# Retention attention and two expert layers on one core: one causal mask, another order of loads, and VectorE's sums moved at the seams

## What is computed

```python
# attention: q, k, v are (4, 8, 768, 64)
for t in range(S):
    state = gamma * state + outer(k[:, :, t], v[:, :, t])
    y[:, :, t] = scale * q[:, :, t] @ state
x = y.transpose(0, 2, 1, 3).reshape(3072, 512)
# first network, w_in 512 x 2048, w_out 2048 x 512
h = x @ w_in
x2 = where(h > 0, h, exp(min(h, 0)) - 1) @ w_out
# second network, w_in 512 x 1024, w_out 1024 x 512
h = x2 @ w_in2
sm = exp(h - max(h)) / (sum(exp(h - max(h))) + 1e-9)
solu = h * sm
out = ((solu - mean) / sqrt(var + 1e-6) * g_ln) @ w_out2
```

## Time and profile before

| | us |
|---|---|
| runs, median of 3 (lowest to highest) | 857.64 (855.99 to 858.91) |
| profiled execution | 856.04 |
| its span | 854.3 |
| TensorE busy in the span | 840.5 |
| VectorE, ScalarE, GpSimd busy | 553.7, 419.0, 390.1 |

### The profile page before, as it was taken

The page is one execution under the profiler, slowest core; times in us unless marked ns, Lnnn a source line. Parts: engine busy times, 40 slices in busy tenths (PEclk is TensorE's granted clock), DMA queues, the critical chain, the costliest instruction groups (busy, mean ns, idle before and its releaser), DMA issues.

```text
span 854.3 us, 12592 instructions
## 1 busy us (share of the span) xinstructions
PE 840.5 (98%) x4852; PEld 694.9 (81%) x4852; DVE 553.7 (65%) x848; ACT 419.0 (49%) x679; POOL 390.1 (46%) x446
## 2 busy tenths in 40 slices
PE   9997999999999999999999999999999999999998
PEld 6987788888888888888888888887878888888886
DVE  3585667677735455576345655788887777777773
ACT  4566665655525555544355565563333333333322
POOL 3577667575006657540256651464253343444200
PEclk9999999999999999999999999999999999999999
DMA  8999611013103001050111101613011111111001
GB/s 305 362 369 347 228 30 45 25 50 128 49 1 96 28 25 49 26 173 1 43 56 31 44 26 44 203 50 98 26 50 50 49 49 39 51 50 50 25 13 50
DMA packets 49359, 73.32 MB, mean 86 GB/s; under 512 B 3218, under 2 KB 23954, under 8 KB 49044
## 3 DMA queue, kind: packets, MB, share of 16 engines
q1 hardware_dynamic: 48864, 72.43, 25.2%
q10 hardware_dynamic: 436, 0.08, 0.0%
HBM read 55.73 MB, written 16.78 MB: 85 GB/s over the span
## 4 chain that ended last, share of the span: by engine, by line
PE 92%; DVE 4%; ACT 1%; issue 1%; POOL 1%; DVEq 0%; ACTq 0%; POOLq 0%
PE ps L673 10%; PE ps L677 10%; PE ps L674 10%; PE ps L626 9%; PE ps L628 9%; PE ps L627 9%; PE ps L783 5%; PE ps L785 5%; PE ps L784 5%; PE ps L685 4%; PE ps L687 4%; PE ps L686 4%; PE ps L576 3%; PE ps L603 3%; PE ps L769 2%; PE ps L589 1%
## 5 line engine op out<-in xcount | busy, mean ns | idle before, releaser
L494 POOL TENSOR_TENSOR u_lo<-u_raw,u_hi 128x256 fp32r<-128x256 f32 x168 | 142.0, 878 | 193.5 <-ACT u_hi L1117 193.5
L673 PE MATMUL ps<-g_hi,wd_hi 128*128 128x512 f32 x384 | 149.4, 389 | 0.0
L674 PE MATMUL ps<-g_hi,wd_lo 128*128 128x512 f32 x384 | 149.4, 389 | 0.0
L677 PE MATMUL ps<-g_lo,wd_hi 128*128 128x512 f32 x384 | 149.4, 389 | 0.0
L626 PE MATMUL ps<-x_hi,u_hi 128*128 128x512 f32 x336 | 131.3, 391 | 1.2 <-DVE u L888 1.2
L627 PE MATMUL ps<-x_hi,u_lo 128*128 128x512 f32 x336 | 130.8, 389 | 0.0
L628 PE MATMUL ps<-x_lo,u_hi 128*128 128x512 f32 x336 | 130.7, 389 | 0.0
L489 POOL TENSOR_TENSOR u_raw<-u_raw 128x256 f32<-128x256 f32 x96 | 88.7, 923 | 17.3 <-DMA u_raw<-w_dram 11.1
L677 PEld LDWEIGHTS ps<-g_lo,wd_hi 128*128 128x128 f32 x384 | 72.1, 188 | 15.0
L674 PEld LDWEIGHTS ps<-g_hi,wd_lo 128*128 128x128 f32 x384 | 72.1, 188 | 15.0
L673 PEld LDWEIGHTS ps<-g_hi,wd_hi 128*128 128x128 f32 x384 | 72.1, 188 | 14.9
(11 more groups left out here) (91 smaller groups left out, 1498.1 us busy)
## 6 DMA issues: line engine op xcount, KB each, us to landing
u_raw<-w_dram SPq DMA_DIRECT2D x24, 512.0 KB, 3.5
k<-units_dram SPq DMA_DIRECT2D x12, 512.0 KB, 6.4
q<-units_dram SPq DMA_DIRECT2D x12, 512.0 KB, 4.8
v<-units_dram SPq DMA_DIRECT2D x12, 512.0 KB, 7.3
x_between<-x SPq DMA_DIRECT2D x24, 256.0 KB, 2.7
x_raw<-x_between SPq DMA_DIRECT2D x12, 512.0 KB, 3.5
out_dram<-y_sb SPq DMA_DIRECT2D x24, 256.0 KB, 2.0
kn<-units_dram SPq DMA_DIRECT2D x10, 512.0 KB, 6.1
```

What stands on the lines that cost most here:

```text
L494: nc.gpsimd.tensor_tensor(u_lo[n % 2][:, o, :], u_raw[n % 2][:, o, :], u_hi[n % 2][:, o, :].bitcast(f32), ALU.subtract).then_inc(ul_done, 1)
L673: nc.tensor.matmul(ps[:, bank + m, :], hi, g_hi[:, no % 3, :], start=(f == 0), stop=False)
L674: nc.tensor.matmul(ps[:, bank + m, :], lo, g_hi[:, no % 3, :], start=False, stop=False)
L677: last = nc.tensor.matmul(ps[:, bank + m, :], hi, g_lo[:, no % 3, :], start=False, stop=(f == NF1 - 1))
```

## The change

1. q is multiplied by its decay in every step. `mask0`, the three row products, the copies out of them and their semaphores are gone; `apply_mask` always takes the causal table. VectorE multiplies the two chunks of q in S0, GpSimd those of all later steps, S6 included.
2. The decay of q comes as a table of 256 KB, first on SyncE's queue; the 7 KB load of rows on ScalarE's queue goes.
3. `load_step(s)` loads q, v, k and natural k of step s, all behind one wait for the attention of step s-3.
4. 13 products on zeros ahead of the first scores, not 6.
5. First network: in pair 0, VectorE's u3 comes ahead of the activation of the first quadrant and the first split of the second weight; u2 of pair 1 comes ahead of pair 0's last activation.
6. Second network: `solu_moments` is cut in two, `solu_spread` and `solu_variance`. u2 of the second pair comes ahead of both for tile 0, u3 ahead of the product of tile 1; u3 of the third pair comes between the two parts of tile 3. For the last pair the maximum of the last tile comes behind the variance of the tile before.

```diff
-WARM = 6
+WARM = 13
             def load_step(s):
-                step_over(s - SLOTS)
+                if s >= SLOTS:
+                    sp.wait_ge(att_done, s - SLOTS + 1)
+                load(s, q_sb, 0, q_in)
                 load(s, v_sb, 3, v_in)
-                if s + 1 < NS:
-                    step_over(s + 1 - SLOTS)
-                    load(s + 1, q_sb, 0, q_in)
+                load(s, k_sb, 1, k_in)
                 if s % NC < NC - 1:
                     load(s, kn_sb, 2, kn_in)
-                if s + 1 < NS:
-                    load(s + 1, k_sb, 1, k_in)
...
-            load(0, k_sb, 1, k_in)
-            load(0, q_sb, 0, q_in)
+            sp.dma_start(q_decay[:, :], tables[:, T_QDEC:T_QDEC + HH * C]).then_inc(q_decay_in, 16)
...
-                if (s + 1) % NC > 0:
+                if s + 1 < NS:
                     decay_q(s + 1)
...
             def scores(s):
-                if s % NC > 0:
-                    pe.wait_ge(q_decayed, decays(s))
-                else:
-                    pe.wait_ge(q_in[slot], 16 * loads(s))
+                if s > 0:
+                    pe.wait_ge(q_decayed, s)
                 for one in range(2):
-                    if s > 0:
+                    if s == 0:
+                        pe.wait_ge(q0_decayed, one + 1)
+                    else:
                         pe.wait_ge(masked, 2 * s - 1 + one)
...
-            spread_row(0, 4)
-            spread_row(1, 5)
...
-                table = causal[:, :].unsqueeze(1).to_broadcast([P, H, C]) if s % NC else mask0
+                table = causal[:, :].unsqueeze(1).to_broadcast([P, H, C])
...
+            dve.wait_ge(q_decay_in, 16)
+            dve.wait_ge(q_in[0], 16)
+            for one in range(2):
+                nc.vector.tensor_tensor(q_sb[0][:, one, :], q_sb[0][:, one, :], q_decay[:, :], ALU.mult)\
+                    .then_inc(q0_decayed, 1)
...
-                dve.wait_ge(p1_kept, n + 1)
-                keep_sum(u2[:, :], n, U2, h21, Y, M6)
-                activate(e11, n, G11, X)
-                if blk == 0:
-                    wd_split_lo(2 * i)
+                if n != 1:
+                    keep_u2(n)
+                if n > 0:
+                    activate(e11, n, G11, X)
+                    if blk == 0:
+                        wd_split_lo(2 * i)
                 keep_sum(u3[:, :], n, U3, h21, Y, M7)
+                if n == 0:
+                    activate(e11, n, G11, X)
+                    wd_split_lo(0)
...
+                if n == 0:
+                    keep_u2(1)
                 activate(stash[:, 2 * i, :], n, G12, stash[:, 2 * i, :])
...
             solu_product(0)
-            solu_moments(0)
             dve.wait_ge(p1_copied, 2)
             add(u2[:, :], 1, U2, kept, Y, P6)
+            solu_spread(0)
+            solu_variance(0)
             solu_normalise(0)
+            add(u3[:, :], 1, U3, kept, Y, P7)
             solu_product(1)
-            add(u3[:, :], 1, U3, kept, Y, P7)
...
-                solu_max(t + 3)
+                if not final:
+                    solu_max(t + 3)
                 solu_product(t + 2)
-                solu_moments(t + 2)
+                solu_spread(t + 2)
+                solu_variance(t + 2)
+                if final:
+                    solu_max(t + 3)
                 solu_normalise(t + 2)
```

More of the change, by code:

```diff
@@ L48, with build @@
 TILE_OF = {place_of(n): n for n in range(NCH)}
-def build(nc, units, w1, w_in2, w_out2, g_ln, tables, rows_table, x_dram, x2_dram, out):
+def build(nc, units, w1, w_in2, w_out2, g_ln, tables, x_dram, x2_dram, out):
     f32, f32r = mybir.dt.float32, mybir.dt.float32r
@@ L863, in split_x_lo @@
                 nc.vector.tensor_tensor(x_lo[:, o], x_raw[:, o], x_hi[:, o].bitcast(f32), ALU.subtract).then_inc(xl_done, 1)
-            for s in range(NS):
[L866 to L874, removed]
+            dve.wait_ge(q_decay_in, 16)
[3 more added lines that the diff above has]
+                    .then_inc(q0_decayed, 1)
+            dve.wait_ge(causal_in, 16)
+            for s in range(NS):
                 apply_mask(s, 0)
@@ L1002, in solu_product, with solu_spread @@
                 nc.vector.tensor_tensor(e3[:, par, :], e3[:, par, :], h2[:, par, :], ALU.mult).then_inc(soft[par], 1)
-            def solu_moments(t):
+            def solu_spread(t):
                 u, par, done = t // 2, t % 2, soft[t % 2]
                 z = SOFT * u
-                esum, esum_eps, r, r2, v = (column(t, n) for n in (2, 3, 4, 5, 7))
+                esum, esum_eps, r = (column(t, n) for n in (2, 3, 4))
                 nc.vector.tensor_scalar(esum_eps, esum, EPS_SM, None, ALU.add).then_inc(done, 1)
@@ L1012, in solu_moments, with solu_variance @@
                     nc.vector.bn_stats(bn[par][:, 6 * q:6 * q + 6], e3[:, par, 512 * q:512 * q + 512]).then_inc(done, 1)
+            def solu_variance(t):
+                u, par, done = t // 2, t % 2, soft[t % 2]
+                z = SOFT * u
+                r, r2, v = (column(t, n) for n in (4, 5, 7))
                 dve.wait_ge(done, z + 7)
@@ L1036, in _ @@
             solu_product(0)
[L1037 removed]
             dve.wait_ge(p1_copied, 2)
             add(u2[:, :], 1, U2, kept, Y, P6)
+            solu_spread(0)
+            solu_variance(0)
             solu_normalise(0)
+            add(u3[:, :], 1, U3, kept, Y, P7)
             solu_product(1)
[L1042 to L1043 removed]
+            dve.wait_ge(soft[1], 3)
             add(h2[:, 1, 512:1024], 1, H22, u3[:, :], W, P5)
             normalised_lo(0)
[L1046 removed]
+            solu_spread(1)
+            solu_variance(1)
             add(h2[:, 1, 0:512], 1, H21, kept, Y, P4)
@@ L1134, in _ @@
             decay_v(0)
-            act.wait_ge(spread, 3)
-            nc.scalar.activation(q_decay[:, :], ps[:, 7, :], ACT.Copy).then_inc(q_decay_made, 1)
             for s in range(NS):
@@ L1319, in decay_tables @@
     state_decay = np.tile(gamma[head] ** C, (1, 2))
-    q_rows = (scale * gamma[:, None] ** (t + 1)[None, :]).reshape(2, HH * C)
-    first, second = np.eye(2)
-    both = np.arange(P) // D == np.arange(2)[:, None]
-    rows = [q_rows, np.tile(first[:, None], (1, P)), np.tile(second[:, None], (1, P)), both]
-    return (np.concatenate([causal, np.eye(P), v_decay, state_decay], axis=1).astype(np.float32),
-            np.concatenate(rows, axis=1).astype(np.float32))
+    q_decay = scale * gamma[head][:, :, None] ** (t + 1)[None, None, :]
+    parts = [q_decay.reshape(P, HH * C), causal, np.eye(P), v_decay, state_decay]
+    return np.concatenate(parts, axis=1).astype(np.float32)
 def kernel(q, k, v, moe_w_in, moe_w_out, moe2_w_in, moe2_w_out, moe2_g_ln):
@@ L1343 @@
         moe_w_out.reshape(NF1, P, DM).transpose(1, 0, 2)], axis=1)
-    tables, rows_table = decay_tables()
     arrays = {
@@ L1350 @@
         "g_ln": np.ascontiguousarray(moe2_g_ln.reshape(NF2, P).T),
-        "tables": tables,
-        "rows": rows_table,
+        "tables": decay_tables(),
     }
```

37 lines of the change are left out of this document (12 added, 25 removed).

## The result

| | before | changed |
|---|---|---|
| median of 8 runs each, us (lowest to highest) | 855.64 (852.47 to 858.91) | 848.18 (846.25 to 849.54) |
| profiled execution, us | 856.04 | 846.25 |
| its span | 854.3 | 844.5 |

The ratio of the runs is 0.9911, with a 95% interval from 0.9890 to 0.9932: the change takes 7.5 us off. The forecast was 850.5, in a range from 846.0 to 855.5. The profiled execution of the change is the fastest of its eight and that of before lies a little above its median, so the two traces differ by 9.8 us and not by 7.5. How much of that is the start's own spread is part of what follows.

What follows compares the result with a forecast made beforehand. TensorE was taken as the bound, its chain stretched or broken in places. From 856.04 us, -3.7 - 1.75 - 0.4 - 0.2 = -6.05 gave 850.0; 0.5 added for the median made 850.5 us, range 846.0 to 855.5.

Steps and rivals of the forecast that it cites:

- The bound: Whole kernel: TensorE is busy 840.5 of 854.3 us; gains lie only where its chain is stretched or broken.
- Term 1: Start of attention: first step at full clock rate, second step starting at 14.3 and not 18.05 us; -3.7 us.
- That the 13 products make the clock: Before the first scores: 13 bf16 products raise TensorE's clock in time; rival, not raised: 853.0 us, chance 0.17.
- Term 2: Attention stalls with each step's loads behind one wait: 3.6 us lost instead of 5.35; -1.75 us, bounds -5.35 and +4.55.
- 1 us lost in S1 and S2 together: Second and third attention steps: instruction blocks stand behind the deep starting queue of loads, about 1 us lost.
- 2.6 us in S8 to S10: Ninth to eleventh attention steps: 2.6 us still lost, as u loads and stores of x still crowd in.
- blocks never late: Rival on the attention stalls: with loads better ordered all 5.35 us go, giving 846.4 us; chance 0.17.
- v late: Tenth attention step, ahead of values: v landing late delayed ScalarE's copy; the 1.29 us break should go.
- The first seam: First network, pairs 0 and 1: VectorE's sums earlier, TensorE then waits for ScalarE's p; -0.4 us, between 0 and -1.2.
- The second seam: Second network: VectorE's sums moved ahead of the statistics delay the normalisation as much; 0, between +0.7 and -1.5 us.
- The last pair: Second network, last pair: last tile's maximum moves behind the variance of the tile before; -0.2 us, between 0 and -0.8.

## Why the prediction was right, and where its terms were not

The direction, the range and the place of the gain were right. By its own steps:

- **The bound.** TensorE's chain, stretched at the start, broken at the end of attention and at the seams. Right: every saving lies there, and nothing moved in between.
- **Term 1, the start, -3.7.** S0 came at 8.24 to 9.57 in three profiles (forecast 9.1), S1 at 13.4 to 15.6 (forecast 14.3). Against the one profile of before that is -2.4 to -4.5. But before's own start was not a constant: over the six profiles that begin as before did (all with the old loads but the one with natural k early, which has 18.72), S1 starts at 15.07 to 17.98, 16.7 on average; over three that begin as the change does (its two, and the one with 17 products), at 14.6. The term is nearer to -2.1, an estimate from few and scattered profiles. The step that failed is that S0's half rate was taken from one profile as the rule.
- **That the 13 products make the clock.** Right in the traces (2.06 against 3.79 us for the scores), though six were enough in two profiles of before, and one of the change lost the clock again in the pause. I priced its absence at 3.0 us, and it was 1.7 in S0, about 1 behind the waits for k, and less than the measurement can tell.
- **Term 2, the losses, -1.75.** This was the mis-sized term: 4.7 us went in the trace (5.34 to 0.66), and 4.7 by the ratio with the loads alone (3.0 to 6.5). "1 us lost in S1 and S2 together" was 0.75 in the first profile, but for k's loads and not for blocks, and nothing in the second; "2.6 us in S8 to S10" was nothing. I had reasoned that a deep queue of loads delays the block. The queue at the start was the deepest, and the block passed 3.3 us after TensorE entered the one before. The prediction also took 6.75 and 9.45 us, from one resumption to the next, as what a block takes; the 9.45 hold the wait for v of 1.29, and the packets themselves passed 4.2 and 7.2 us after TensorE entered the block before, with some 2.4 more until it resumed. And the three breaks stood 6, 5 and 3 matmuls into the group, not 5 to 7. The rival "blocks never late" was the true case there, and the sentence of the Trainium skill (*Runtime: NRT & Kernel Launch*, instruction fetch mechanics) that crossing a block is mostly hidden held for the new order, as it had not for the old.
- **v late.** Right, and larger than the 1.29 us that I gave it: in the old order v and natural k are late by turns.
- **The first seam, -0.4.** -0.5, and by the path forecast: TensorE now waits for ScalarE's p, 0.83 us.
- **The second seam, 0.** +0.3: the sums moved ahead delayed the normalisation and n_lo, and TensorE waits 1.4 and 1.3 us for them. Within its bounds.
- **The last pair, -0.2.** -0.3.

Put together, -2.1 for the start (average of traces), -4.7 for the loads (by the runs) and -0.5 for the seams (one trace each) make -7.3, and -7.5 was measured. That the forecast of -7.1 (850.5 against 857.64) came so near is in part luck: the start was taken too large and the loads too small, and 1.1 of the 7.1 is no term of the sum but what lay between the profiled execution and the median of three runs. The median of before over eight runs is 855.64, 2.0 us lower, which makes up most of the 2.3 us between 850.5 and 848.18.

Why the block comes late in the old order stays open. It is not the depth of the queue alone, since the new order has that too. Natural k a step earlier brought the packets to 2.9 to 3.2 us after the entry and made the breaks inside the key-value groups of S8 to S10 vanish; with the stores held back the packet of 7.2 us passed after 5.9. What ties a packet of instructions to the place of a load, no run shows.

## What to carry to other kernels

When two operands of the same step are each just late, one of them moved alone can give nothing, and only both together show the gain; a test of single parts would have thrown this change away. When TensorE stops where the program has no wait, look in the trace for the packet of the instruction queue just ahead of where it goes on. On an in-order engine a late load costs what stands behind its consumer (here the copy of the step before), so load first what feeds the longest queue, and all of a step behind one wait as early as its slot allows. And profile the kernel before twice: a start that depends on the clock can differ by 3 us between two executions.

## What the runs showed of the hardware

- A pause of 1.5 to 2.6 us ahead of S0 or inside it is sometimes followed by half rate and sometimes not: the granted clock fell behind 1.55 us (before, second profile), 1.61 us (v of S9 ahead of wd) and 2.31 us (change, second profile), and stayed at full behind 1.50 us (change), 1.78 us (change, old loads) and 2.56 us (17 products).
- The moment at which the clock rises differs between executions of the same start: behind six bf16 products TensorE was at full rate at once in two of eight profiles, during S0 in two, and at about 17 us in four. With 13 or 17 products it was at full rate before S0 in all four.
- The granted clock in the rows read 1.00 in S0 of before's first profile and of the one with 6 products, where score matmuls took 417 ns instead of 272; in the second profiles it read 0.50 for the same durations. The column can't be trusted ahead of the first change of level.
- A packet of TensorE's instructions (0.02 MB) passed 2.2 to 3.5 us after TensorE had entered the block before, at S7 to S10, wherever natural k was loaded a step earlier; with natural k in its old place it took up to 7.2. Data traffic stood at 98.8% and 105.2% of the 16 engines while such a packet was awaited in S9 (before, change). TensorE resumed 2.2 to 2.6 us behind the packet in 16 of 16 breaks.
